# Attention and two dense layers: normalisation moved to the dense layer's input, operand splits moved to GpSimd

## The chip, the cores and the metric

The kernel runs on one core of a Trainium2 chip. A core has five engines with queues of their own: TensorE (PE in the profile; matrix products into PSUM), VectorE (DVE), ScalarE (ACT), GpSimd (POOL, which reads and writes SBUF alone) and SyncE (SP), which here issues most DMAs. The metric is the device time of the program in microseconds, lower is better.

## The reference

Block-causal attention over 4 batches x 8 heads, 576 positions, 64 channels a head, then two dense layers on 2,304 tokens of 512 channels with 2,048 hidden ones. All is float32.

```python
scores = scale * np.matmul(q, k.transpose(0, 1, 3, 2))      # scale 1/8
mask = block_i >= block_j                                   # blocks of 64 positions
scores = np.where(mask, scores, -1e9)
scores = scores - np.max(scores, axis=-1, keepdims=True)
attn = np.exp(scores)
attn = attn / (np.sum(attn, axis=-1, keepdims=True) + 1e-09)
x = np.matmul(attn, v)                                      # heads side by side: (2304, 512)
h = x @ w_in;  g = h * np.clip(h + 3.0, 0.0, 6.0) / 6.0;  x = g @ w_out
h = x @ w_in2; g = h * np.tanh(softplus(h));              out = g @ w_out2
```

## The kernel before

**Float32 in two parts.** A float32 operand x is written as hi, x stored as float32r (the format that TensorE takes at its fast rate), and lo = x - hi, stored as float32r too. A product is then two or three float32r matmuls. Making hi is a copy on some engine, making lo a subtraction of two tensors.

**A head.** q, k and v of head n are loaded by SP (`load_qk`, `load_v`), two buffers each, q and k twice, into both halves of the partitions. ScalarE makes hi of k (`split_k_hi`, L588), VectorE hi and lo of the scaled q (`split_q_hi` L781, `split_q_lo` L786) and hi and lo of v (L842, L850), GpSimd lo of k (L976). The scores of a head are five row tiles i = 0 to 4, of 128, 256, 384, 512 and 576 columns (`scores(s, i)`, L405 with hi of k, L410 with lo; L408 adds the mask to the last 64 columns; tile 0 is computed 256 wide). For each tile VectorE takes the negative row maximum (`row_max`, L792, L796), ScalarE the exponential with the row sum (`exps`, L599), VectorE the reciprocal of the sum (L799), and GpSimd multiplies the tile by it (`normalise`, L969). Then TensorE transposes the tile in 128 x 128 pieces (`prob_transposes(s, u)`, L423, four groups u = 0 to 3 in four PSUM banks), ScalarE copies the transposed pieces out as hi (`split_probs_hi`, L605 to L609) and VectorE makes lo (`split_probs_lo`, L802). Group 0 and a corner of group 3 stay in full float32 (`pt32`). `attend(s, half)` (L443) multiplies with v, [hi | lo] of v being the stationary operand: half 0 gives the first 256 positions from `pt32`, half 1 the other 320. ScalarE copies the result to SBUF (`copy_o`, L614), and SP stores it to `attn_t` in DRAM (`store_o`, L294).

**Order.** Every engine runs a list of its own, written out by hand in `attention_step`: a step works on head n, the scores of n + 1 and the q and k of n + 2. Steps 2 to 23 run in a hardware loop of two steps, the others are unrolled. Engines wait on semaphores alone.

**The seam.** `EARLY_ADD`, `EARLY_X` and `EARLY_W` name the steps in which first pieces of the dense layer are prepared: four chunks c of the first x block (`add_x` on GpSimd, L994, adds the two halves of the product; `split_x_hi` on ScalarE; `split_x_lo` on GpSimd, L998) and weight tiles 0 to 3 (`split_w_hi` on ScalarE, L670, `split_w_lo` on VectorE, L860). All four chunks are ready by step 29; SP has loaded weight tiles 4 and 5 as well (`load_w`, 512 KB each, two buffers `wraw`). In the last step TensorE puts `h_matmuls` of hidden tiles 0 and 1 between the parts of head 31 to fill its waits; then `dense_block` takes hidden tile f + 3 (`h_matmuls`) and output step f (`y_matmuls`) in turn. `h_matmuls(f)` of the first block waits for weight tile f, and the first one for all x chunks.

Of the kernel before, what the change touches and what calls it, by code (L numbers as in the profile page):

```python
# [5 lines left out]
ALU = mybir.AluOpType  # L21
# [34 lines left out]
PT_COLS = P * (4 * 4 + 4) + TAIL  # L56

PT, PL, ST, AV = 4, 3, NT, 2
FIRST, LOOP_FROM, LOOP_TO = -2, 2, NHEAD - 8


def build(nc, qk, v_main, v_tail, w, w2, out):
    ctx = ExitStack()
    with ctx:
# [8 lines left out]
        x2_t = nc.dram_tensor("x2_t", (D, TOK), F32).ap()  # L73

# [4 lines left out]
        xraw = [sb(f"xraw{s}", [P, 2, TB], F32) for s in range(2)]  # L79
# [20 lines left out]
        rowsum = [sb(f"rowsum{s}", [P, NT], F32) for s in range(2)]  # L100
        rinv = [sb(f"rinv{s}", [P, NT], F32) for s in range(2)]

        with ExitStack() as att:
# [10 lines left out]

            pt32 = [ab(f"pt32{s}", [P, 3 * P + TAIL], F32) for s in range(2)]
# [21 lines left out]

        q_hi = sem("q_hi")
# [9 lines left out]
        rinv_ready = sem("rinv_ready")  # L148
        probs_ready = sem("probs_ready")
# [4 lines left out]
        p_lo = sem("p_lo")  # L154

# [8 lines left out]
        x_added = sem("x_added")  # L164
        x_hi = sem("x_hi")
# [51 lines left out]
        def count(step, ahead, m, c):  # L217

            g, par = step
            return g * (2 * m) + ((par + ahead) * m + c)  # L220

        def slot(step, ahead):
            return (step[1] + ahead) % 2

        def has(step, ahead):

            g, par = step
            return not isinstance(g, int) or 0 <= 2 * g + par + ahead < NHEAD

        def pairs(step, ahead):  # L230

            g, par = step
            return g + ((par + ahead) // 2 + 1)

        def steps(n0, n1):
            return [(n // 2, n % 2) for n in range(n0, n1)]

        SCORE_BANK = (0, 2, 0, 1, 2)
        PT_BANK = (3, 4, 5, 6)
# [8 lines left out]
        def early(table, step):  # L253

            g, par = step
            return table.get(2 * g + par, ()) if isinstance(g, int) else ()


        def pt_source(u):

            w = P if u < 3 else TAIL
            return bank(PT_BANK[u], (u + 2) * w).rearrange("p (j q) -> p j q", q=w)[:, 0:min(u + 2, 4), :]

        def pt_part(t, u):

            i = u + 1
            if i < 4:
                return t[:, i * P:i * P + (i + 1) * 4 * P].rearrange("p (j q) -> p j q", q=4 * P)[:, :, 0:P]
            return t[:, 4 * P:20 * P].rearrange("p (j q) -> p j q", q=4 * P)[:, :, 0:TAIL]
# [3 lines left out]
        def _(sp):  # L273
            def load_qk(step, ahead):

                if has(step, ahead - 2):
                    sp.wait_ge(q_lo, count(step, ahead - 2, 1, 1))
                    sp.wait_ge(k_lo, count(step, ahead - 2, 1, 1))
                s, n = slot(step, ahead), count(step, ahead, 1, 0)
                for half in range(2):  # L280
                    sp.dma_start(qkin[s][half * DH:(half + 1) * DH, :, :], qk[n, :, :, :]).then_inc(qk_loaded[s], 16)

            def load_v(step, ahead):
                if has(step, ahead - 2):
                    sp.wait_ge(v_split, count(step, ahead - 2, 1, 1))
# [17 lines left out]
            def load_x(layer, blk, c):  # L303

                if not (blk == (0, None) and c < 2):
                    sp.wait_ge(x_lo, lin(blk, DC, c - 1))
# [755 lines left out]
```

## Time and profile before

| | |
|---|---|
| time, median of 3 runs | 1075.72 us (1075.23 to 1076.01) |
| span of the profiled execution, first to last instruction | 1073.4 us |
| TensorE busy | 1026.8 us, 96% |
| VectorE busy | 723.4 us, 67% |
| ScalarE busy | 551.4 us, 51% |
| GpSimd busy | 266.0 us, 25% |
| mean granted TensorE clock | 0.996 of full |

The profiled execution has no time of its own beside its span; the runs of the table were timed separately. Busy shares are means over a kernel with two very different parts, the attention (up to about 265 us) and the dense layers. A group of instructions lists busy time, mean length in ns and the idle time of the engine ahead of it with the engine that ended it. Lengths of instructions back to back on VectorE overlap a little, so a sum of lengths is more than the busy time.

### The profile page before, as it was taken

Reading aid. Unit: us, or ns where it says so; the run is one execution under the profiler, and the core shown is the slowest. Engines: PE = TensorE matmul, PEld = TensorE weight load, DVE = VectorE, ACT = ScalarE, POOL = GpSimd, SP = SyncE. Lnnn points to the kernel's source line nnn. Section 1 sums busy time; section 2 is a strip of 40 time slices with the busy share of each in tenths; the row PEclk is TensorE's granted clock in tenths of the full one; section 3 lists DMA queues with packets and bytes.
Section 4 is the critical chain, followed back from the end, with each engine's and each line's share of the span. In section 5 each row is a group of like instructions: output and inputs, shape, how many; then the busy total and the mean of one; then the engine's idle time right before and its main releaser. Section 6 shows DMA issues by size and latency. Waiting matters only on the chain.

```text
span 1073.4 us, 18142 instructions
## 1 busy us (share of the span) xinstructions
PE 1026.8 (96%) x5760; PEld 952.7 (89%) x5760; DVE 723.4 (67%) x1468; ACT 551.4 (51%) x1257; POOL 266.0 (25%) x275
## 2 busy tenths in 40 slices
PE   4889898988999999999999999999999999999998
PEld 3777777778999999999999999898999989999896
DVE  5999999995732223222232356988988889888886
ACT  5777787876632223222232345655555555555553
POOL 3777777795210202002020010010100001000000
PEclk9999999999999999999999999999999999999999
DMA  6656555652621101111011143200001000010000
GB/s 183 177 133 143 129 145 135 171 146 73 194 69 45 45 1 59 29 44 44 0 59 54 51 134 127 68 16 30 24 7 44 15 29 23 6 44 0 30 1 30
DMA packets 38087, 73.92 MB, mean 69 GB/s; under 512 B 7072, under 2 KB 23456, under 8 KB 38048
## 3 DMA queue, kind: packets, MB, share of 16 engines
q1 hardware_dynamic: 32000, 63.98, 21.9%
q10 hardware_dynamic: 6048, 9.44, 2.4%
q8 instruction: 22, 0.36, 0.1%
q14 instruction: 17, 0.14, 0.0%
HBM read 54.53 MB, written 18.87 MB: 68 GB/s over the span
## 4 chain that ended last, share of the span: by engine, by line
PE 75%; DVE 16%; issue 6%; POOL 1%; ACT 1%; DMA 0%; DVEq 0%; SPq 0%
PE psum L534 36%; PE psum L511 12%; PE psum L510 12%; PE psum L509 12%; DVE negmax L792 3%; DVE qs L786 2%; DVE wlo_early L802 2%; DVE rinv L799 1%; DVE ptlo L802 1%; DVE negmax L796 1%; DVE qs L781 1%; DVE vs L842 1%; DVE vs L850 1%; PE psum L443 1%; POOL klo L976 1%
## 5 line engine op out<-in xcount | busy, mean ns | idle before, releaser
L998 POOL TENSOR_TENSOR xlo<-xraw,xhi 128x384 f32 (+1 forms) x48 | 58.7, 1222 | 640.8 <-ACT xhi L679 640.8
L906 DVE SCALAR_TENSOR_TENSOR gbuf<-ebuf,psum 128x384 f32<-128x384 f32 x96 | 53.1, 553 | 230.5 <-ACT ebuf L731 230.5
L731 ACT ACTIVATE ebuf<-psum,three 128x384 f32<-128x384 f32 x96 | 55.8, 581 | 246.4 <-PE psum L511 246.4
L969 POOL TENSOR_TENSOR prob<-prob,rinv 128x128 f32<-128x128 f32 (+4 forms) x160 | 140.1, 892 | 62.7 <-DVE rinv L799 62.7
L511 PE MATMUL psum<-xhi,wlo_late 128*128 (+1 forms) x384 | 129.9, 338 | 0.0
L510 PE MATMUL psum<-xlo,whi_late 128*128 (+1 forms) x384 | 129.8, 338 | 0.0
L509 PE MATMUL psum<-xhi,whi_late 128*128 (+1 forms) x384 | 129.5, 337 | 0.0
L509 PE MATMUL psum<-xhi,whi_early 128*128 (+1 forms) x384 | 128.7, 335 | 0.0
L511 PE MATMUL psum<-xhi,wlo_early 128*128 (+1 forms) x384 | 128.7, 335 | 0.0
L510 PE MATMUL psum<-xlo,whi_early 128*128 (+1 forms) x384 | 128.5, 335 | 0.0
L704 ACT ACTIVATE ghi<-gbuf 128x384 fp32r<-128x384 f32 x192 | 100.1, 522 | 54.8 <-DVE gbuf L927 53.5
L873 DVE SCALAR_TENSOR_TENSOR glo<-gbuf,ghi 128x384 fp32r<-128x384 f32 x192 | 121.9, 635 | 4.2 <-ACT ghi L704 3.6
L599 ACT ACTIVATE prob<-psum,negmax 128x128 f32<-128x128 f32 (+4 forms) x160 | 91.2, 572 | 51.0 <-DVE negmax L796 37.7
L405 PE MATMUL psum<-khi,qs 128*128 128x256 f32 (+2 forms) x192 | 75.5, 398 | 40.9 <-ACT prob L599 24.1
L738 ACT ACTIVATE late<-ebuf,two 128x384 f32<-128x384 f32 x96 | 59.2, 616 | 87.9 <-DVE ebuf L890 87.8
L405 PEld LDWEIGHTS psum<-khi,qs 128*128 128x128 f32 x192 | 37.9, 197 | 51.6 <-ACT prob L599 29.1
L423 PE MATMUL psum<-ident,prob 128*128 128x128 f32 x480 | 73.7, 279 | 0.5 <-POOL prob L969 0.5
L510 PEld LDWEIGHTS psum<-xlo,whi_late 128*128 128x128 f32 x384 | 72.1, 188 | 2.3
L509 PEld LDWEIGHTS psum<-xhi,whi_late 128*128 128x128 f32 x384 | 72.1, 188 | 2.1
L510 PEld LDWEIGHTS psum<-xlo,whi_early 128*128 128x128 f32 x384 | 72.1, 188 | 2.0
L509 PEld LDWEIGHTS psum<-xhi,whi_early 128*128 128x128 f32 x384 | 72.1, 188 | 1.9
L410 PE MATMUL psum<-klo,qs 128*128 128x256 f32 (+2 forms) x192 | 72.9, 385 | 0.0
(92 smaller groups left out, 2587.3 us busy)
## 6 DMA issues: line engine op xcount, KB each, us to landing
qkin<-in_qk SPq DMA_DIRECT2D x64, 288.0 KB, 4.3
wraw<-in_w SPq DMA_DIRECT2D x32, 512.0 KB, 3.4
attn_t<-late SPq DMA_DIRECT2D x64, 144.0 KB, 2.4
xraw<-attn_t SPq DMA_DIRECT2D x24, 384.0 KB, 3.3
x_t<-ystage ACTq DMA_DIRECT2D x24, 192.0 KB, 1.9
xraw<-x_t SPq DMA_DIRECT2D x24, 192.0 KB, 2.4
out<-ystage ACTq DMA_DIRECT2D x18, 256.0 KB, 2.1
vin<-in_v_main SPq DMA_DIRECT2D x32, 128.0 KB, 2.5
```

What stands on the lines that cost most here:

```text
L405: pe.matmul(bank(pb, w), q_tile, khi[s][:, k0:k0 + w], start=True, stop=False)
L410: last = pe.matmul(bank(pb, w), q_tile, klo[s][:, k0:k0 + w], start=False, stop=True)
L423: last = pe.transpose(bank(PT_BANK[u], P, c0), prob[s][:, POFF[i] + j * P:POFF[i] + (j + 1) * P], ident[:, :])
L509: pe.matmul(bank(f % HB, TB), hi, x_part(xhi, blk, c), start=(c == 0), stop=False)
L510: pe.matmul(bank(f % HB, TB), hi, x_part(xlo, blk, c), start=False, stop=False)
L511: last = pe.matmul(bank(f % HB, TB), lo, x_part(xhi, blk, c), start=False, stop=(c == DC - 1))
L534: last = pe.matmul(bank(4 + c, Y_COLS[layer]), stat, mov, start=(f == 0 and m == 0), stop=(f == FT - 1 and m == 2), skip_group_check=True)
L599: nc.scalar.activation(dst, src, ACT.Exp, bias=negmax[s][:, i:i + 1], accum_out=rowsum[s][:, i:i + 1]).then_inc(exp_done, 1)
L704: nc.scalar.activation(ghi[f % GS][:, :], gbuf[f % 2][:, :], ACT.Copy, scale=(1.0 / 6.0 if layer == 0 else 1.0)).then_inc(g_hi, 1)
L738: nc.scalar.activation(rbuf[f % 2][:, :], ebuf[f % 2][:, :], ACT.Ln, bias=two[:, 0:1]).then_inc(ln_ready, 1)
L873: nc.vector.scalar_tensor_tensor(out=glo[f % GS][:, :], in0=gbuf[f % 2][:, :], scalar=(1.0 / 6.0 if layer == 0 else 1.0), in1=ghi[f % GS][ ...
L969: nc.gpsimd.tensor_tensor(p, p, rinv[s][:, i:i + 1].to_broadcast([P, w]), ALU.mult).then_inc(probs_ready, 1)
```

## The change

1. **Normalisation.** The probabilities stay unnormalised. Row sums of the eight heads of a batch are gathered in one tile; at the end of a batch TensorE transposes it (`turn_sums`), VectorE takes the reciprocals (`invert_sums`), SP stores them to DRAM (`store_rinv`, five DMAs). `load_x` of the first dense layer fetches with every x chunk the reciprocals, each row broadcast to 64 partitions (two more DMAs), and `add_x` gets a second operation on GpSimd that multiplies by them.
2. **q, k, v on GpSimd.** It scales q in place, makes hi of k, q and v by copies, and lo of q, v and k by subtractions, for q and k three heads ahead. ScalarE and VectorE no longer touch them. `copy_o` moves from ScalarE to VectorE.
3. **Transposed probabilities.** All are kept in two float32r parts; `pt32` goes. `attend` is 2 matmuls of 128 columns in half 0 and 10 of 448, 320, 192 and 64 columns in half 1. Score tile 0 is computed 128 wide.
4. **Order.** Everything is unrolled from step -3, with a new interleaving, other PSUM banks for the scores (two pairs by the parity of the head) and other steps for the early work; SP loads weight tiles 2 and 3 at step 4 and tile 4 only after the last stores.

```diff
-PT_COLS = P * (4 * 4 + 4) + TAIL
+PT_ROW = SEQ - P
+PT_COLS = (NT + 1) * PT_ROW
+PT_ORDER = (0, 1, 3, 2)
+FIRST = -3
...
-        EARLY_ADD = {NHEAD - 8: (0,), NHEAD - 7: (1,), NHEAD - 5: (2,), NHEAD - 4: (3,)}
-        EARLY_X = {NHEAD - 7: (0,), NHEAD - 6: (1,), NHEAD - 4: (2,), NHEAD - 3: (3,)}
-        EARLY_W = {-2: (0, 1), -1: (2, 3)}
+        EARLY_ADD = {NHEAD - 5: 0, NHEAD - 4: 1, NHEAD - 3: 2, NHEAD - 2: 3}
+        EARLY_X = {NHEAD - 4: 0, NHEAD - 3: 1, NHEAD - 2: 2, NHEAD - 1: 3}
+        EARLY_W = {-2: 0, -1: 1, NHEAD - 2: 2, NHEAD - 1: 3}
...
+            def store_rinv(b):
+                sp.wait_ge(rinv_ready, b + 1)
+                for i in range(NT):
...
+                    sp.dma_start(r_d[:, t0 + i * P:t0 + i * P + w], rinv[i * HEADS:(i + 1) * HEADS, 0:w]
+                                 ).then_inc(rinv_stored, 16)
...
+                    for h in range(2):
+                        sp.dma_start(x[h * DH:(h + 1) * DH, 2, :],
+                                     r_d[2 * c + h:2 * c + h + 1, tokens].to_broadcast([DH, TB])
...
+                if in_use(n):
+                    store_o(n)
+                    if n % HEADS == HEADS - 1:
+                        store_rinv(n // HEADS)
+            for f in range(4, FT):
...
                 load_w(0, f)
+            attention_stored(BATCH)
...
             def attend(n, half):
...
+                    parts = [(0, 0, t[s][:, 0:P]) for t in (pthi, ptlo)]
...
+                    parts = [(j, max(j - 1, 0) * P, pt_row(t[s], j, max(j, 1) * P))
+                             for j in range(NT) for t in (pthi, ptlo)]
...
             def attention_step(n):          # TensorE
+                last_step = n == NHEAD - 1
+                if in_use(n + 1):
+                    scores(n + 1, 2)
+                if in_use(n):
+                    prob_transposes(n, 3)
+                if in_use(n + 1):
+                    scores(n + 1, 3)
+                if in_use(n):
+                    prob_transposes(n, 2)
                 if last_step:
                     h_matmuls((0, None), 0)
+                if in_use(n + 1):
+                    scores(n + 1, 4)
+                if in_use(n):
+                    attend(n, 0)
                 if last_step:
                     h_matmuls((0, None), 1)
+                if in_use(n + 2):
+                    scores(n + 2, 0)
+                if in_use(n + 1):
+                    prob_transposes(n + 1, 0)
+                    prob_transposes(n + 1, 1)
+                if in_use(n + 2):
+                    scores(n + 2, 1)
+                if in_use(n):
+                    attend(n, 1)
+                    if n % HEADS == HEADS - 1:
+                        turn_sums(n // HEADS)
...
+            def attention_step(n):          # VectorE
+                if in_use(n):
+                    split_probs_lo(n, 3)
+                    copy_o(n, 0)
+                    split_probs_lo(n, 2)
+                if in_use(n + 1):
+                    row_max(n + 1, 4)
+                if in_use(n + 2):
+                    row_max(n + 2, 0)
+                if in_use(n + 1):
+                    split_probs_lo(n + 1, 0)
+                if in_use(n + 2):
+                    row_max(n + 2, 1)
+                if in_use(n):
+                    copy_o(n, 1)
+                if in_use(n + 2):
+                    row_max(n + 2, 2)
+                if in_use(n + 1):
+                    split_probs_lo(n + 1, 1)
+                if in_use(n + 2):
+                    row_max(n + 2, 3)
+                if n in EARLY_W:
+                    split_w_lo(0, EARLY_W[n])
+                if in_use(n) and n % HEADS == HEADS - 1:
+                    invert_sums(n // HEADS)
...
+            def attention_step(n):          # GpSimd
+                if in_use(n + 3):
+                    scale_q(n + 3)
+                    split_k_hi(n + 3)
+                    split_q_hi(n + 3)
+                if in_use(n + 1):
+                    split_v_hi(n + 1)
+                if in_use(n + 3):
+                    split_q_lo(n + 3)
+                if in_use(n + 1):
+                    split_v_lo(n + 1)
+                if in_use(n + 3):
+                    split_k_lo(n + 3)
+                if n in EARLY_ADD:
+                    add_x((0, None), EARLY_ADD[n])
+                if n in EARLY_X:
+                    split_x_lo(0, (0, None), EARLY_X[n])
...
                 nc.gpsimd.tensor_tensor(x[:, 0, :], x[:, 0, :], x[:, 1, :], ALU.add).then_inc(x_added, 1)
+                pool.wait_ge(x_added, lin(blk, DC, c + 1))
+                nc.gpsimd.tensor_tensor(x[:, 0, :], x[:, 0, :], x[:, 2, :], ALU.mult).then_inc(x_scaled, 1)
```

## Rows read from the trace of the kernel before

**Rows 1.** Head of the page of the profile.

```profile
span 1073.4 us, 18142 instructions
```

**Rows 2.** Windows: length, busy us (count) of PE, PEld, DVE, ACT, POOL; clock, DMA.

```profile
60.00:210.60 150.60, 134.34 (x905) 113.28 (x902) 149.34 (x341) 118.75 (x361) 114.76 (x121) 1.00 0.59 142
...
248.00:251.00 3.00, 2.77 (x11) 2.70 (x12) 0.82 (x4) 1.15 (x5) 2.77 (x5) 0.53 0.03 5
...
300.00:400.00 100.00, 100.00 (x573) 100.00 (x572) 28.10 (x52) 28.90 (x57) 10.57 (x10) 1.00 0.12 38
```

**Rows 3.** Groups by line, VectorE, 60 to 210.6 us (20 heads).

```profile
L792 DVE TENSOR_REDUCE negmax<-psum 128x1 f32<-128x256 f32 (+1 forms) x80 | 36.5, 477 | 0.0
...
L781 DVE TENSOR_SCALAR qs<-qkin 128x576 fp32r<-128x576 f32 x21 | 25.6, 1219 | 0.0
...
L786 DVE SCALAR_TENSOR_TENSOR qs<-qkin,qs 64x576 fp32r<-64x576 f32 x20 | 25.1, 1256 | 0.6
...
L799 DVE RECIPROCAL rinv<-rowsum 128x1 f32<-128x1 f32 x100 | 15.3, 153 | 0.6
...
L802 DVE TENSOR_TENSOR ptlo<-psum,pthi 128x384 fp32r<-128x384 f32 (+2 forms) x30 | 14.7, 544 | 0.0
...
L850 DVE TENSOR_TENSOR vs<-vin,vs 128x320 fp32r<-128x320 f32 x20 | 13.7, 683 | 0.0
...
L842 DVE CAST vs<-vin 128x320 fp32r<-128x320 f32 x20 | 9.3, 465 | 0.0
```

**Rows 4.** Groups by line, GpSimd, 60 to 210.6 us.

```profile
L969 POOL TENSOR_TENSOR prob<-prob,rinv 128x512 f32<-128x512 f32 (+4 forms) x101 | 89.5, 902 | 35.8 <-DVE rinv L799 35.8
...
L976 POOL TENSOR_TENSOR klo<-qkin,khi 128x576 fp32r<-128x576 f32 x20 | 28.1, 1406 | 0.0
```

**Rows 5.** Groups by form, GpSimd, 0 to 30 us.

```profile
L969 POOL TENSOR_TENSOR prob<-prob,rinv 128x576 f32<-128x576 f32 x1 | 1.1, 1141 | 0.0
...
L1014 POOL TENSOR_SCALAR_AFFINE_SELECT ident<-ident 128x128 f32<-128x128 f32 x1 | 0.3, 292 | 0.2 <-POOL two L1012 0.2
...
L1008 POOL MEMSET ident<- 128x128 f32 x1 | 0.2, 204 | 0.3 <-POOLq L1049 0.3
...
L1011 POOL MEMSET three<- 128x1 f32 x1 | 0.1, 98 | 0.0
```

**Rows 6.** Timeline, VectorE, before GpSimd is at work.

```profile
6.08 0.46 DVE L781 TENSOR_SCALAR qs<-qkin 128x576 fp32r<-128x576 f32 x1 [4.03 <-DMA qkin<-in_qk]
```

**Rows 7.** Timeline, TensorE: start us, length us; brackets: idle time, releaser.

```profile
27.77 0.41 PE L443 MATMUL psum<-whi_early,vs 128*128 128x320 f32 x1
...
40.71 0.81 PE L443 MATMUL psum<-pt,vs 128*128 128x256 f32 x4
...
42.34 0.38 PE L405 MATMUL psum<-khi,qs 128*128 128x256 f32 x1 [0.81 <-ACT prob L599]
...
248.23 0.55 PE L405 MATMUL psum<-khi,qs 128*128 128x256 f32 x1 [2.28 <-POOL klo L976]
...
262.62 0.42 PE L509 MATMUL psum<-xhi,whi_early 128*128 128x384 f32 x1
...
264.79 0.31 PE L443 MATMUL psum<-pthi,vs 128*128 128x320 f32 x1
...
266.13 0.34 PE L509 MATMUL psum<-xhi,whi_early 128*128 128x384 f32 x1
...
270.43 0.44 PE L534 MATMUL psum<-ghi,whi_early 128*128 128x384 f32 x1
```

**Rows 8.** Timelines of ScalarE, VectorE, SP; DMA issues of the weight tiles.

```profile
272.88 1.06 ACT L670 ACTIVATE whi_early<-wraw 128x1024 fp32r<-128x1024 f32 x1 [1.99 <-DMA wraw<-in_w]
...
273.97 1.23 DVE L860 TENSOR_TENSOR wlo_early<-wraw,whi_early 128x1024 fp32r<-128x1024 f32 x1 [1.53 <-ACT whi_early L670]
...
266.79 1.12 SPq L294 DMA_DIRECT2D attn_t<-late  x2
...
wraw<-in_w SPq DMA_DIRECT2D x32, 512.0 KB, 3.4
```

More of the change, by code:

```diff
@@ L272, in _, with pt_row @@
+            if u == 0:
+                return rows[:, 0:3, 0:P]
+            return rows[:, 1:u + 3, u * P:u * P + (P if u < 3 else TAIL)]
+        def pt_row(t, j, q0):
+            return t[:, PT_ROW * (j + 1) + q0 - P:PT_ROW * (j + 2)]
         @block.sync
         def _(sp):
[L274 to L279, printed above, removed]
-                for half in range(2):
-                    sp.dma_start(qkin[s][half * DH:(half + 1) * DH, :, :], qk[n, :, :, :]).then_inc(qk_loaded[s], 16)
@@ L283, in load_v, with load_qk @@
[L283 to L295 removed]
+            def load_qk(n):
+                if in_use(n - 2):
+                    sp.wait_ge(q_lo, n - 1)
+                    sp.wait_ge(k_lo, n - 1)
+                for half in range(2):
+                    sp.dma_start(qkin[n % 2][half * DH:(half + 1) * DH, :, :], qk[n, :, :, :]
+                                 ).then_inc(qk_loaded[n % 2], 16)
@@ L323, in _ @@
-            for step in steps(-2, LOOP_FROM):
-                load_qk(step, 4)
-                if has(step, 1):
-                    load_v(step, 3)
-                if not has(step, 1):
+            load_qk(0)
+            load_w(0, 0)
+            load_qk(1)
+            load_v(0)
+            load_w(0, 1)
+            load_v(1)
+            for n in range(FIRST, NHEAD):
+                if 2 <= n + 5 < NHEAD:
+                    load_qk(n + 5)
+                if 2 <= n + 3 < NHEAD:
+                    load_v(n + 3)
+                if n == 4:
@@ L328, in _ @@
                     load_w(0, 2)
                     load_w(0, 3)
-                if has(step, 0):
-                    store_o(step, 0, step[1])
-            load_w(0, 4)
-            load_w(0, 5)
-            with sp.Fori(LOOP_FROM // 2, LOOP_TO // 2) as g:
-                batch, pair = sp.snap(g // (HEADS // 2)), sp.snap(g % (HEADS // 2))
-                for par in range(2):
-                    load_qk((g, par), 4)
-                    load_v((g, par), 3)
-                    store_o((g, par), batch, pair * 2 + par)
@@ L494, in attention_step @@
-                if has(step, 0):
-                    pe.wait_ge(p_lo, count(step, 0, PL, 3))
-                    attend(s0, 1)
+                if in_use(n + 2):
[9 more added lines that the diff above has]
+                        turn_sums(n // HEADS)
```

500 lines of the change are left out of this document (196 added, 304 removed).

## The prediction

> **What bounds the kernel now.** The profiled execution spans 1073.4 us [rows 1]; the median of the runs is 1075.7, so 2.3 us lie around the span, and I carry them over unchanged. I read the stretches first. In a stretch of dense work TensorE is busy for all of its 100 us [rows 2], and I take the dense layers to be like it throughout: no helper engine sets their time. In the attention loop (20 heads in 150.6 us, 7.53 us a head) it is another picture: VectorE is busy for 149.3 of the 150.6 us, TensorE for 134.3, GpSimd 114.8, ScalarE 118.8 [rows 2]. So VectorE sets the period of the 32 heads, and TensorE pays with one gap of about 0.8 us a head, waiting for an exponential that waits for a row maximum [rows 7]. Next comes VectorE's own list [rows 3] and GpSimd's [rows 4], since the change empties the first and fills the second. Last the seam between attention and dense layer [rows 7, 8]. Measured from the first second-half `attend` (27.77) to the last (264.79) less the two `h_matmuls` put between (2.17 each, as the one from 262.62), the 31 periods take 237.0 - 4.3 = 232.7 us [rows 7].
>
> **VectorE.** Removed per head: the two q splits (25.6/21 + 25.1/20 = 2.48), five reciprocals (0.77), the v cast and v remainder (0.47 + 0.68): 4.4 us. Kept: four row maxima (36.5/20 = 1.83) and the fifth, of 576 columns (0.74, an estimate from the remainder's 0.54 for 384), and three remainders (0.54 each) [rows 3]. Added: a remainder of 384 columns (0.54), 64 columns more in the tail's (0.07), two copies out of PSUM of 128 and 448 columns (about 0.28 and 0.61, as PSUM reads of such width in these rows). Sum 5.7 us as listed, an upper bound, since back-to-back instructions overlap a little in the records. VectorE is no longer the bound.
>
> **ScalarE** was busy for 5.9 us a head [rows 2]. It loses the k cast and both copies of the output, keeps the exponentials and gets no new operation in the loop (the first transposed tile becomes float32r, the tail's two copies one), so it stays under 5.9 and is not the bound.
>
> **GpSimd.** Removed: five normalisations, 89.5/20 = 4.5 us a head. Kept: k remainder, 1.41 [rows 4]. Added: `scale_q`, `split_k_hi`, `split_q_hi` (one input, 576 columns), `split_v_hi` (one input, 320), `split_q_lo` (two inputs, 576 columns on half of the partitions; the time goes by columns, 1.4), `split_v_lo` (two inputs, 320: 1.41 x 320/576 and a fixed part, 0.87). Nothing in the trace is a one-input copy or scale on GpSimd. Bounds for 576 columns: from below the memsets, 0.10 for one column and 0.20 for 128, so 0.8 ns a column, 0.10 + 0.45 = 0.56; from above the multiply with a broadcast operand that the profile has undisturbed, 1.14. The one op with one tensor input, the select that makes the identity, took 0.29 for 128 columns: 0.19 above the one-column memset, 1.5 ns a column, 0.96 at 576 [rows 5]. I take 0.90, nearest to that row, and 0.53 for 320 columns. Sum: 3 x 0.90 + 0.53 + 2 x 1.41 + 0.87 = 6.9, less 0.04 overlap for each of seven, 6.65; by the bounds 5.6 and 7.4. The Trainium skill says of GpSimd (GPSIMD Engine Reference, 4.1 Engine selection) that one-input ops run roughly at line rate; by that, an estimate of 0.5 plus a fixed 0.15, the head would cost GpSimd about 5.9. The same page (8. Key points) calls VectorE about twice as fast for elementwise work, which speaks against moving the splits; no run here has the one-input case.
>
> GpSimd did not run free before: with it busy, VectorE's `split_q_hi` took 1.22 us [rows 3], alone 0.46 [rows 6]. After the change every VectorE operation of the loop reads PSUM, with at most one operand in SBUF, the kind that kept its 0.54 us beside a busy GpSimd [rows 3]. So I add no contention. The Trainium skill has the rule (SBUF — State Buffer, Who interferes with whom): VectorE contends with GpSimd in two-port modes or with two SBUF inputs, not otherwise; the pair 0.46 and 1.22 agrees.
>
> **TensorE.** A head holds 7.53 less the gap of 0.8, 6.7 us of matmuls, of it 0.2 the end of the last one ahead of the gap: 6.5. `attend` took about 0.6 for 384 columns in full float32 (0.8 with its end) and 1.34 for the second half (264.79 to 266.13) [rows 7]. Now it is twelve float32r matmuls with 3,200 columns (2 x 128 in the first half; 4 x 448, 2 x 320, 2 x 192, 2 x 64 in the second). One `h_matmuls`, twelve float32r matmuls of 384 columns, takes 2.17 us [rows 7], 0.47 ns a column, so 1.5 for all; the narrow ones cannot follow each other quite so fast, and I take 1.7 against 1.94. The first score tile is 128 wide, not 256: 256 columns less, -0.1. That gives 6.1 us. But matmuls in float32r under 256 columns (128, 192, 64 and the 128-wide scores, 768 + 256 columns a head) do not occur before. The bound from above: they cost what full float32 costs, 0.81 us for 384 columns [rows 7]; with 0.2 taken off for the end of the last one, 1.6 ns each, so 1,024 x (1.6 - 0.47) ns = 1.2 us more, less the allowance for narrow ones: 7.2 us. I take the float32r row, the nearest in kind.
>
> **Period.** GpSimd's 6.65 is the longest of the sums as taken, before TensorE's 6.1, ScalarE's under 5.9 and VectorE's 5.7. Each head has to go through TensorE, ScalarE and VectorE in turn, and I add 0.15 for waits between engines this close: 6.8. The new order gives each chain (scores, maximum, exponential, transpose, split, remainder) half a head or more before TensorE asks for it, and q, k and v are made up to three heads ahead, so I find no chain of the loop longer than the period. SP gets no new DMA inside a batch; its loads of q and k wait for GpSimd's remainders two heads back and land in 4 us, under a head. 31 x 6.8 = 210.8: -21.9 us.
>
> **Start.** GpSimd now makes q and k of head 0 in five operations one after another, 3 x 0.9 + 2 x 1.4 = 5.5 us against 2.7 before, but two of the four early weight splits leave ScalarE's and VectorE's start (1.06 and 1.23 each [rows 8]). I count 0, bounds -2 and +3.
>
> **Seam.** Two new waits. First, the last early x chunk is now split in the last step, after `prob_transposes(31, 2)`: ScalarE's split of 512 columns of probabilities and of 384 of x (0.6 and 0.5, from its 1.06 for 1,024), GpSimd's remainder (1.0 for 384 columns, by the 1.41 for 576 [rows 4]), and the hand-overs 0.1: `h_matmuls(0)` stands 2.2 us on TensorE, and behind it, in order, both halves of `attend`. Second, SP: weight tiles 4 and 5 were loaded ahead, so TensorE had no gap from 262.62 to the first y at 270.43 (two `h_matmuls` of 2.17 after `attend`) [rows 7]. Now `load_w(0, 4)` stands behind `store_o(31)` and `store_rinv(3)`. From the end of the last `attend`: copy and inversion about 0.6, seven issues at 0.56 (two took 1.12), issue and landing of the tile 3.4, ScalarE 1.06, VectorE 1.23 [rows 8]: about 10.2 us. TensorE has h(2), h(3) and y(0) to do, 3 x 2.17: it waits 3.7 us for tile 4. Such gaps have a second price: after 2.28 us of idleness the 3 us from 248 ran at a granted clock of 0.53, the 1.2 GHz level [rows 2, 7], where work takes twice its time: +1.5 us a gap. Against that, part of the first gap only takes the place of waits that the last step had before. I take the two waits as 5.6 (of 5.9) and the clock as 0.7: seam +6.3. With no new wait it would be 0; with both at the lower clock and slower small loads, 10.
> The store of the inverses, the broadcast loads and the extra multiply (one of 1.0 us for each of 24 chunks) lie in the dense layer beside TensorE's full load, where GpSimd is busy a tenth of the time [rows 2]; four batch ends add a 128-column transpose and a reciprocal of some 0.3 us, hidden. If that cover went, 24 us.
>
> **Sum.** 1073.4 - 21.9 + 0 + 6.3 + 2.3 = 1060 us.
>
> **Rivals.**
> A. Copies on GpSimd near memset rate (0.7 an operation or less, so GpSimd at most 5.9) and narrow float32r at full rate: 6.1 a head, bound by TensorE, 189.1 - 232.7 + 6.3: 1038, and 1032 if TensorE's sum is too high by 0.2. For it: the memset rows [rows 5]. Against: no tensor is read in them. The line-rate rule of the Trainium skill named above would give this case.
> B. Narrow float32r costs like float32: TensorE 7.2 a head, 223.2 us, -9.5 + 6.3: 1072. For it: full float32 at 1.6 against 0.47 ns a column shows how much a fall-back would cost. Against: no row shows one.
> C. The other side: one-input operations cost what the broadcast multiply does, 1.14, or more. GpSimd then needs 7.4 a head, 7.5 with the waits between engines, as much as VectorE needed before; the loop gives back nothing, and the seam stays: 1082. It decides from a period of 7.3, where the loop's gain equals the seam: GpSimd at 7.15, an operation at 1.04. At 1.41, the two-input price, a head takes 8.6 and the kernel 1116.
> D. The loop is as said and the seam costs nothing, the new waits hidden by work that moves up: 1054.
>
> **Chances.** As said, with D (1052 to 1066): 0.46. A: 0.17. B: 0.15. C: 0.22, of it 0.04 within 0.2% of before (2.2 us, about what a measurement of this kernel can tell from no change). Faster 0.78, same 0.04, slower 0.18. A range of 1032 to 1084 leaves out the far ends of A and C; the likeliest case by itself has 1052 to 1067.
>
> **What would show it.** GpSimd busy above 0.9 in the loop, VectorE near 0.75; heads 6.8 us apart; the three 576-column operations near 0.9; TensorE's waits on `q_lo`/`k_lo`; a gap of 2 us before the first `h_matmuls`, one of 4 before h(4), ended by a weight remainder. It is wrong if a one-input operation takes over 1.04 us, if matmuls of 64 to 192 columns take more than 0.15, or if GpSimd's q and k come late for the scores although it has idle time.

## The result and the profile after

The changed kernel takes 1082.05 us (median of 6 runs, 1079.91 to 1084.32), the kernel before 1075.87 on the same chip (6 runs, 1073.87 to 1078.49): ratio 1.0056, 95% interval 1.0041 to 1.0071. It is slower by 0.6%; the forecast was 1060 and faster. The profiled execution spans 1082.5 us, is the longest of the six (1084.32 by its own time) and ran at a mean granted clock of 0.982 (before: 0.996), so a ledger made on it has 9.1 us to explain where the medians differ by 6.2.

The head of the page after, with its busy shares and the chain that ended last by engine:

```profile
span 1082.5 us, 16881 instructions
...
PE 1012.1 (94%) x5700; PEld 947.0 (87%) x5700; DVE 661.9 (61%) x1278; ACT 511.4 (47%) x1129; POOL 331.0 (31%) x331
...
PE 77%; POOL 11%; issue 5%; DVE 3%; DMA 3%; SPq 1%; ACT 0%; POOLq 0%; DVEq 0%
```

The same chain before:

```profile
PE 75%; DVE 16%; issue 6%; POOL 1%; ACT 1%; DMA 0%; DVEq 0%; SPq 0%
```

GpSimd has taken VectorE's place on the chain, and 3% of it are now DMAs. The windows after, with the columns of [rows 2], answer to them; the stretch from 100 to 150 and two short ones are added:

```profile
60.00:210.00 150.00, 125.58 (x877) 110.26 (x875) 110.00 (x227) 95.37 (x285) 139.93 (x143) 0.98 0.58 149
100.00:150.00 50.00, 42.24 (x301) 37.00 (x300) 37.53 (x78) 32.62 (x98) 47.94 (x50) 1.00 0.58 145
72.00:76.00 4.00, 0.00 (x0) 0.00 (x0) 0.92 (x3) 0.05 (x1) 3.71 (x6) 0.83 0.96 253
76.00:80.00 4.00, 3.97 (x14) 3.53 (x15) 2.26 (x5) 1.64 (x6) 2.99 (x2) 0.50 0.35 94
...
300.00:400.00 100.00, 100.00 (x579) 100.00 (x578) 33.45 (x55) 32.08 (x61) 22.34 (x21) 1.00 0.23 71
```

From 100 to 150 GpSimd is busy for 47.94 of 50 us and nobody else is near: the loop is bound where the forecast put it. But the second-half `attend` of successive heads starts every 7.20 us, not every 6.8. GpSimd's forms after say why (60 to 210 us; busy, mean ns, idle before):

```profile
L881 POOL TENSOR_SCALAR qkin<-qkin 128x576 f32<-128x576 f32 x20 | 33.2, 1658 | 0.0
L903 POOL TENSOR_TENSOR qs<-qkin,qs 64x576 fp32r<-64x576 f32 x21 | 29.8, 1417 | 3.2 <-POOL vs L917 2.6
L909 POOL TENSOR_TENSOR klo<-qkin,khi 128x576 fp32r<-128x576 f32 x21 | 29.6, 1409 | 0.0
L923 POOL TENSOR_TENSOR vs<-vin,vs 128x320 fp32r<-128x320 f32 x21 | 18.3, 873 | 3.0
L888 POOL CAST qs<-qkin 128x576 fp32r<-128x576 f32 x20 | 13.5, 675 | 0.0
L894 POOL CAST khi<-qkin 128x576 fp32r<-128x576 f32 x20 | 13.4, 670 | 4.0 <-PE psum L397 4.0
L917 POOL CAST vs<-vin 128x320 fp32r<-128x320 f32 x20 | 9.2, 461 | 0.0
```

The seven means sum to 7.16 us. In 100 to 150 GpSimd is busy for 6.90 us a head (47.94/50 of 7.20): back-to-back instructions overlap by about 0.04 each in the records, and the other 0.29 us of the period are two waits of GpSimd on itself. `split_q_lo` (L903) and `split_v_lo` (L923) each wait for a semaphore that the instruction right before them in GpSimd's own list raises: 3.2 us in 21 and 3.0 in 21, 0.15 and 0.14 a head. The three remainders are as forecast (1.42, 1.41, 0.87). The casts are cheaper than the 0.90 and 0.53 taken: 0.67 and 0.46. The scaling of q in place (L881) is far dearer: 1.66, more than a subtraction with two inputs.

The short windows show a second loss. In 72 to 76 TensorE does nothing and the DMA engines are 0.96 busy; in 76 to 80 it works at 0.50, the 1.2 GHz level. SP's queue and VectorE's timeline around that place, after:

```profile
64.89 0.47 SPq L262 DMA_DIRECT2D vin<-in_v_tail  x1
65.39 1.06 SPq L289 DMA_DIRECT2D wraw<-in_w  x2
66.50 1.27 SPq L268 DMA_DIRECT2D attn_t<-late  x2
```

```profile
75.08 0.29 DVE L743 COPY late<-psum 128x128 f32<-128x128 f32 x1 [6.16 <-DMA attn_t<-late]
75.29 0.68 DVE L734 TENSOR_TENSOR wlo_early<-psum,whi_early 128x512 fp32r<-128x512 f32 x1
75.89 0.75 DVE L729 TENSOR_REDUCE negmax<-psum 128x1 f32<-128x576 f32 x1
```

In step 4 SP issues two weight tiles (1 MB) and then `store_o(4)`. The second half of the store lands at 74.99, 8.0 us after its issue; in the other steps a half takes 3.1 (median). `copy_o(6)` wants the stage buffer of head 4, so it stands on VectorE for 6.16 us, and behind it, in order, stand the remainder of the probabilities (L734) and the row maximum (L729), for which TensorE and ScalarE wait in turn. At step 26 VectorE waits in the same way, 4.70 us up to 236.16, but for another reason: six DMAs of the x chunks stand ahead of `store_o(26)`, and SP needs 3.5 us to issue them. The store then lands 3.9 us after its own issue, not 8. SP's queue there, after:

```profile
227.98 0.52 SPq L298 DMA_DIRECT2D xraw<-attn_t  x1
...
231.50 1.23 SPq L268 DMA_DIRECT2D attn_t<-late  x2
```

TensorE's waits at the seam, after, and ScalarE's queue there (the counterparts of [rows 7, 8]):

```profile
261.82 0.69 PE L485 MATMUL psum<-xhi,whi_early 128*128 128x384 f32 x1 [4.31 <-POOL xlo L954]
...
280.79 0.69 PE L510 MATMUL psum<-ghi,whi_early 128*128 128x384 f32 x1 [5.93 <-DVE glo L794]
```

```profile
277.49 1.06 ACT L616 ACTIVATE whi_early<-wraw 128x1024 fp32r<-128x1024 f32 x1 [10.88 <-DMA wraw<-in_w]
278.45 0.56 ACT L677 ACTIVATE ebuf<-psum,three 128x384 f32<-128x384 f32 x1
278.92 0.51 ACT L650 ACTIVATE ghi<-gbuf 128x384 fp32r<-128x384 f32 x1
```

The first wait is for x chunk 3. Its buffer is freed by the remainder of chunk 1 only at 253.4, the chunk and its reciprocals land at 257.7, then four GpSimd operations of 1.0 follow: the chunk's two, and behind them the remainders of chunk 2 and of chunk 3. After the wait TensorE works at the 1.2 GHz level: the granted clock is 0.52 in 262 to 266, and `h_matmuls(0)` takes 4.0 us (261.82 to 265.83) instead of 2.17. GpSimd's timeline, after:

```profile
257.80 0.99 POOL L948 TENSOR_TENSOR xraw<-xraw 128x384 f32<-128x384 f32 x1 [3.11 <-DMA xraw<-r_d]
258.87 0.99 POOL L950 TENSOR_TENSOR xraw<-xraw 128x384 f32<-128x384 f32 x1
259.82 1.95 POOL L954 TENSOR_TENSOR xlo<-xraw,xhi 128x384 fp32r<-128x384 f32 x2
```

The second wait is not at h(4), as forecast, but at the first `y_matmuls`: ScalarE's queue holds `split_w_hi(4)` ahead of `split_g_hi` of the first hidden tile, and stands in it for 10.88 us until the late tile 4 has landed.

Where the time went, in the profiled executions (marks: start of second-half `attend` of head 0, of head 31, first `y_matmuls`, end; before: 27.77, 264.79, 270.43, 1073.4 [rows 1, 7]; after: 28.71, 268.14, 280.79, 1082.5):

| part | after less before, us |
|---|---|
| start, up to head 0 | +0.9 |
| 31 periods of 7.20 for 7.506 | -9.5 |
| heads 6 to 9 take 32.9 for 28.8 (store behind two weight tiles) | +4.1 |
| heads 28 to 30 take 25.0 for 21.6 (store behind six x DMAs, x work) | +3.4 |
| last step, 16.1 for 7.2 + 4.3 (wait for x chunk 3) | +4.6 |
| last `attend` to the first y, 12.65 for 5.64 (weight tile 4) | +7.0 |
| dense layers | -1.3 |
| sum (remainder -0.1 to the spans' +9.1) | +9.2 |

The last step is set against a full period and the two `h_matmuls`. But the last heads have less to do: where all early work is done ahead (e6 below) heads 30 and 31 take 5.46 and 7.45 us, the two `h_matmuls` included. Against that the waits of the last step cost 8.7 us, not 4.6.

### The profile page after: what moved, and what is told of

It is laid out like the page before. It is cut to its first block, busy times and chain, and to the rows that moved or that the text cites. A ratio compares the mean times of both kernels' runs of the same rounds, so it can differ in the third digit from the quotient of the medians.

```text
span 1082.5 us, 16881 instructions
## 1 busy us (share of the span) xinstructions
PE 1012.1 (94%) x5700; PEld 947.0 (87%) x5700; DVE 661.9 (61%) x1278; ACT 511.4 (47%) x1129; POOL 331.0 (31%) x331
## 4 chain that ended last, share of the span: by engine, by line
PE 77%; POOL 11%; issue 5%; DVE 3%; DMA 3%; SPq 1%; ACT 0%; POOLq 0%; DVEq 0%
PE psum L510 36%; PE psum L485 12%; PE psum L487 12%; PE psum L486 12%; POOL qkin L881 3%; POOL qs L903 3%; PE psum L435 2%; POOL vs L923 2%; POOL qs L888 1%; PE psum L415 1%; DMA xraw<-r_d 1%; PE psum L397 1%; PE psum L392 1%; POOL vs L917 1%; DMA attn_t<-late 1%
## 5 line engine op out<-in xcount | busy, mean ns | idle before, releaser
L392 PE MATMUL psum<-khi,qs 128*128 128x128 f32 (+2 forms) x192 | 73.0, 385 | 38.3 <-issue 24.0
L725 DVE TENSOR_REDUCE negmax<-psum 128x1 f32<-128x128 f32 (+3 forms) x128 | 62.3, 486 | 22.1 <-PE psum L397 18.8
L487 PEld LDWEIGHTS psum<-xhi,wlo_early 128*128 128x128 f32 x384 | 72.9, 190 | 0.0
```

Source lines behind the costliest of these rows:

```text
L392: pe.matmul(bank(pb, w), q_tile, khi[s][:, k0:k0 + w], start=True, stop=False)
L487: last = pe.matmul(bank(f % HB, TB), lo, x_part(xhi, blk, c), start=False, stop=(c == DC - 1))
L725: nc.vector.reduce_max(negmax[s][:, i:i + 1], bank(b, PW[i]), AX.X, negate=True).then_inc(max_ready, 1)
```

## Experiments

Each run of a kernel of its own is set against runs of the kernel before on the same chip, as a ratio with a 95% interval. "Period" is the distance of second-half `attend`s in steps without extra work. Four suspects: the scaling operation, the store behind the weight tiles, the x chunks, weight tile 4.

**e1, stores first.** In each step SP issues `store_o` ahead of the weight tiles and of the x chunks of the first block; nothing else is changed.

```diff
+                if in_use(n):
+                    store_o(n)
                 if n == 4:
                     load_w(0, 2)
                     load_w(0, 3)
...
-                if in_use(n):
-                    store_o(n)
```

> Only SP's order differs from the changed kernel: in steps 4, 26, 28 and 29 the store of the head's output is issued before the two weight tiles and the x chunks, not behind them. Theory 1 (the store of head 4 and head 26 lies in the DMA queues behind 1 MB of other loads, and copy_o two heads later waits for its buffer): the two long periods of 11.6 and 10.1 us fall to about 7.2, and the periods around them lose their slow-clock tail; the span falls by 6 to 7.5 us, to about 1075. Rival (the DMA engines are simply full there, whoever comes first): the wait moves to the loads of q, k, v of the next heads, GpSimd idles, and less than 3 us come back.

Measured: 1080.41 us, ratio 1.0053 (1.0037 to 1.0070), span 1078.1. Heads 6 to 9 are back at 7.20 each: the store behind the weight tiles is shown as the cause there. At the x chunks the wait only moved. GpSimd's and TensorE's timelines of this kernel:

```profile
229.62 1.01 POOL L948 TENSOR_TENSOR xraw<-xraw 128x384 f32<-128x384 f32 x1 [2.09 <-DMA xraw<-r_d]
230.71 0.99 POOL L950 TENSOR_TENSOR xraw<-xraw 128x384 f32<-128x384 f32 x1
231.67 1.65 POOL L881 TENSOR_SCALAR qkin<-qkin 128x576 f32<-128x576 f32 x1
```

```profile
233.79 0.69 PE L392 MATMUL psum<-khi,qs 128*128 128x384 f32 x1 [3.16 <-ACT prob L574]
```

The x DMAs, now issued later, are late for `add_x`; GpSimd stands, ScalarE's x split waits for it with the exponentials behind, and TensorE waits 3.16 us. Head 29 takes 11.7 us and the last step 18.0 instead of 16.1. So the expectation held for one half: the span fell by 4.4 us, not by 6 to 7.5, and the median by 1.6.

**e2, weights ahead.** Weight tiles 2 and 3 are split in steps 8 and 10 instead of 30 and 31, which frees their buffers, and tiles 4 and 5 are loaded in step 12.

```diff
-        EARLY_W = {-2: 0, -1: 1, NHEAD - 2: 2, NHEAD - 1: 3}
+        EARLY_W = {-2: 0, -1: 1, 8: 2, 10: 3}
+                if n == 12:
+                    load_w(0, 4)
+                    load_w(0, 5)
...
-            for f in range(4, FT):
+            for f in range(6, FT):
```

> Weight tiles 2 and 3 are split in steps 8 and 10 instead of 30 and 31, and SP loads tiles 4 and 5 in step 12, behind the store. Theory 1 (the 5.9 us gap ahead of the first y is the load of tile 4, which SP issues only after the last stores, and ScalarE's queue stands behind its split): the gap goes, with its slow-clock tail; 6 to 8 us less than the changed kernel, about 1075. Rival (the gap belongs to the store of the reciprocals and the wait for the inverted sums ahead of the dense block): it stays at 5 us or more, and less than 2 us come back.

Measured: 1074.63 us (10 runs), ratio 0.9989 (0.9974 to 1.0004), span 1075.7. TensorE's timeline of this kernel at the seam:

```profile
263.88 0.69 PE L488 MATMUL psum<-xhi,whi_early 128*128 128x384 f32 x1 [6.24 <-POOL xlo L957]
...
276.65 0.34 PE L513 MATMUL psum<-ghi,whi_early 128*128 128x384 f32 x1
```

The first y has no wait any more: from the last `attend` (270.84) to it 5.81 us instead of 12.65, which is [rows 7]'s 5.64 again. Some of the 6.8 is paid back in the loop (heads 9 and 11 take 7.7 and 8.2, the wait for chunk 3 is 6.24 for 4.31), some more is won in the dense layers (2.7 us). Against the changed kernel the medians give -7.4 us, as expected. The late weight tile is shown as the cause of the wait at the first y, and its price there is the ledger's. Heads 9 and 11 show a price of weight splits in the loop. VectorE's and GpSimd's timelines of this kernel:

```profile
95.21 1.97 DVE L784 TENSOR_TENSOR wlo_early<-wraw,whi_early 128x1024 fp32r<-128x1024 f32 x1
```

```profile
96.07 2.62 POOL L884 TENSOR_SCALAR qkin<-qkin 128x576 f32<-128x576 f32 x1
```

VectorE's remainder of a weight tile, with both inputs in SBUF, runs for 1.97 us where it takes 1.22 elsewhere, and GpSimd's scaling beside it for 2.62 instead of 1.66. The same happens again at 110 us.

**e3, scaling on ScalarE.** `scale_q(n + 4)` goes to ScalarE, behind `exps(n + 1, 3)`, as one activation; GpSimd keeps the rest.

```diff
-                nc.gpsimd.tensor_scalar(q, q, SCALE, None, ALU.mult).then_inc(q_scaled, 1)
+                nc.scalar.activation(q, q, ACT.Copy, scale=SCALE).then_inc(q_scaled, 1)
```

> The scaling of q (1.66 us a head on GpSimd) is done by ScalarE in place, with one Copy with scale, a step ahead; nothing else moves. Theory 1 (GpSimd's sum is the period of the loop): GpSimd needs 5.5 us a head, TensorE becomes the bound at 6.2 to 6.5, 0.7 to 1.0 us a head less: 22 to 31 us less than the changed kernel, 1051 to 1060. Rival (the chain of TensorE, ScalarE and VectorE is as long as the period already): less than 5 us.

Measured: 1129.49 us, ratio 1.0498 (1.0479 to 1.0516), span 1127.6. The expectation failed badly. The waits of this kernel in 60 to 210 us (total, times, longest):

```profile
POOL khi L898 <- PE psum L397: 61.3, 12, 7.5
...
PE psum L392 <- ACT prob L579: 39.4, 9, 4.9
ACT qkin L562 <- DMA qkin<-in_qk: 36.0, 8, 4.9
```

The scaling itself costs ScalarE 0.68 us. But the q and k of head n + 4 are loaded only when GpSimd has used up those of n + 2, and they had not landed; ScalarE stood up to 4.9 us in the scaling with the exponentials behind it, TensorE waited for them, GpSimd waited for the scores, and so loaded later still. Heads alternate between 11.3 to 13.9 and about 5.8 us, and over 60 to 210 us the granted clock is 0.85.

**e4, scaling as a multiply with a broadcast operand.** The same shape in place, but as the two-input operation with a one-column tile of 1/8.

```diff
-                nc.gpsimd.tensor_scalar(q, q, SCALE, None, ALU.mult).then_inc(q_scaled, 1)
+                nc.gpsimd.tensor_tensor(q, q, eighth[:, 0:1].to_broadcast([P, SEQ]), ALU.mult).then_inc(q_scaled, 1)
```

> GpSimd keeps the scaling, but as a multiply of two tensors whose second is one broadcast column, the form that took 1.14 us for 576 columns before. Theory 1 (GpSimd bounds the loop, and its tensor_scalar is slow as an instruction, not because it writes in place): the operation takes 1.14 instead of 1.66, the period 6.7 instead of 7.2, 15 to 16 us less: about 1066. Rival (in-place work over the whole tile is what costs, in any form): it takes about 1.66 again and the time is that of the changed kernel, within 3 us.

Measured: 1069.32 us, ratio 0.9940 (0.9923 to 0.9957), span 1069.7. The operation takes 1.15 us, the period is 6.67, as expected. The stalls are at the same places as in the changed kernel, and in the loop and the last step longer: head 6 takes 12.8 us (VectorE's wait for the store is 7.42 for 6.16), and heads 6 to 9, heads 28 to 30 and the last step stand 7.3, 4.3 and 5.4 us above the period, where they stood 4.1, 3.4 and 4.6. These 4.9 us account for the shortfall: 12.7 us came back, and not 15 to 16. With this one line the change is faster than before, by 0.6%. The operation's row in this kernel:

```profile
L882 POOL TENSOR_TENSOR qkin<-qkin,eighth 128x576 f32<-128x576 f32 x21 | 24.1, 1149 | 1.4 <-DMA qkin<-in_qk 1.4
```

**e5, scaling on ScalarE, later.** As e3, but `scale_q(n + 3)`, behind `exps(n + 1, 1)`.

> As the run before with the scaling of q on ScalarE, but asked for a head later in ScalarE's queue (head n + 3 in step n, behind the exponential of tile 1), so that the load has landed when ScalarE comes to it. Theory 1 (the 12 us periods of that run come from ScalarE's queue standing behind a load that waits, through the two buffers, for GpSimd; GpSimd's sum is still what bounds the changed kernel): periods of 6.2 to 6.6, the rest of the ledger as in the changed kernel, 22 to 31 us less than it: 1051 to 1060. Rival (two q and k buffers can't feed a loop shorter than 7 us, or the chain of TensorE, ScalarE and VectorE is as long): 7.0 us or more a head, above 1072.

Measured: 1053.61 us (1050.79 to 1059.31), ratio 0.9796 (0.9750 to 0.9842), span 1054.4, inside the expected 1051 to 1060. Periods go from 5.65 to 7.5, 6.3 on average from head 10 to head 27. ScalarE still waits for loads in the scaling, 8.3 us in all from 100 to 150 and 2.3 at most at once, but no longer long enough to start the alternation. The stalls at head 6 and at the seam are there as before.

**e6, the work of the seam ahead.** Stores first; weight tiles 2 to 5 loaded one at a time in steps 4, 6, 19, 21 and tiles 2, 3 split in 8 and 10; the four x chunks loaded in 11, 13, 16, 18, added in 14, 16, 20, 22 and split a step later; the next block's two in the last steps. GpSimd keeps its 1.66 us scaling.

```diff
-        EARLY_ADD = {NHEAD - 5: 0, NHEAD - 4: 1, NHEAD - 3: 2, NHEAD - 2: 3}
-        EARLY_X = {NHEAD - 4: 0, NHEAD - 3: 1, NHEAD - 2: 2, NHEAD - 1: 3}
-        EARLY_W = {-2: 0, -1: 1, NHEAD - 2: 2, NHEAD - 1: 3}
+        EARLY_ADD = {14: 0, 16: 1, 20: 2, 22: 3}
+        EARLY_X = {15: 0, 17: 1, 21: 2, 23: 3}
+        EARLY_W = {-2: 0, -1: 1, 8: 2, 10: 3}
+        LOAD_W = {4: 2, 6: 3, 19: 4, 21: 5}
+        LOAD_X = {11: 0, 13: 1, 16: 2, 18: 3}
```

> Scaling as in the changed kernel. Stores first in each step of SP; weight tiles 2 to 5 one at a time in steps 4, 6, 19 and 21; x chunks one at a time in steps 11 to 18, made in steps 14 to 23; so none of this is left for the end. Theory 1 (the ledger: 4.1 us at heads 6 to 9, 3.4 at 28 to 30, 4.6 in the last step, 7.0 between the last attend and the first y): all four go, and GpSimd, the bound, pays for 12 us of x work in the loop: 1082 - 19 + 8 to 12, so 1071 to 1075. Rival (these gaps are one mechanism's symptoms and come back elsewhere): above 1078.

Measured: 1070.62 us, ratio 0.9955 (0.9938 to 0.9971), span 1067.6, just under the expected 1071 to 1075. Every stall of the ledger is gone: head 6 at 7.19, last step 7.45 with both `h_matmuls`, 5.8 from the last `attend` to the first y. But steps with early work take up to 10.2 us. Heads 16 to 24 come to 12.0 us above 7.2 a head, the 12 x 1.0 us of GpSimd that the four chunks need; heads 9 to 12, beside the two weight splits, come to 2.0, and two GpSimd operations there are 1.0 us longer than usual, as in e2. Where GpSimd sets the period, its x work is paid in full.

**e7 and e8, both remedies together.** e6's schedule with e4's multiply, and with e5's scaling on ScalarE.

> Work ahead, and q scaled on GpSimd by the broadcast multiply. Theory 1: 0.53 us a head less than the run with work ahead alone, -16: 1055 to 1060. Rival: as soon as the loop is shorter, ScalarE and VectorE chains bound it, less than 8 us less.

> Work ahead, and q scaled by ScalarE where the load has landed. GpSimd has 5.5 us a head, TensorE 6.2: x work on GpSimd is hidden. Theory 1: periods 6.2 to 6.5, no gaps at the end, 1036 to 1046. Rival: ScalarE or the chain bounds at 7: above 1060.

Measured: e7 1054.08 us, ratio 0.9801 (0.9779 to 0.9823), period 6.67; e8 1036.57 us, ratio 0.9635 (0.9607 to 0.9662), span 1034.5, periods 5.65 to 8.2; e7 is 1 us under what was expected, e8 at its lower end. Against the changed kernel e4 saves 12.7 us, e6 11.4 and both together 28.0, 3.9 more than the sum. The ledgers have a reason for it: the faster loop of e4 made the stalls 4.9 us longer, and in e7 they are not there. The medians alone, from several chips, would not settle a difference of this size.

**e9, a copy in place.** The changed kernel with the scaling replaced by a copy onto the same place; the scaling is left out.

```diff
-                nc.gpsimd.tensor_scalar(q, q, SCALE, None, ALU.mult).then_inc(q_scaled, 1)
+                nc.gpsimd.tensor_copy(q, q).then_inc(q_scaled, 1)
```

> The changed kernel with GpSimd's scaling of q replaced by a plain copy onto the same place, same shape (so q stays unscaled: the scaling by 1/8 is left out). It tells apart two reasons for the 1.66 us: that the operation writes where it reads, or that it is arithmetic with a constant instead of a copy. Theory (the kind of instruction): the copy in place takes 0.67 us like the two casts, GpSimd's list falls from 7.16 to about 6.2 a head, the loop is then bound by TensorE or near it at about 6.3 (31 x 0.9 less, so a span near 1056 with the stalls of the changed kernel left in). Rival (writing in place): the copy takes about 1.6 too and the span stays at 1080.

Measured: 1052.51 us, ratio 0.9792 (0.9769 to 0.9815), span 1049.7, period 6.18. The row of this kernel:

```profile
L881 POOL COPY qkin<-qkin 128x576 f32<-128x576 f32 x23 | 15.3, 664 | 0.0
```

0.66 us, with tensor and place unchanged: it is not the writing in place that costs 1.66, it is the operation with a constant. GpSimd's list is now 6.17 us, and the period 6.18: from 100 to 200 us GpSimd has no idle time but the two short waits on itself, so it still sets the period, and not TensorE, as had been expected.

**e10, no scaling of q.** e6's schedule; the exponential takes the scale 1/8, and VectorE multiplies each negated row maximum by 1/8.

```diff
-                nc.scalar.activation(dst, src, ACT.Exp, bias=negmax[s][:, i:i + 1],
+                nc.scalar.activation(dst, src, ACT.Exp, scale=SCALE, bias=negmax[s][:, i:i + 1],
+                nc.vector.tensor_scalar(negmax[s][:, i:i + 1], rawmax[s][:, i:i + 1], SCALE, None, ALU.mult
+                                        ).then_inc(max_ready, 1)
```

> The schedule of e8, but q is not scaled at all: the exponential takes scale 1/8, and VectorE multiplies each negated row maximum by 1/8 (an operation of 128x1, five a head). GpSimd's list is then 5.5 us a head, ScalarE has no operation that waits for a load, and VectorE gets five small operations of about 0.1 to 0.15 us (0.5 to 0.75 us on a list of 5.4). Theory: the loop is bound by TensorE, 6.1 to 6.4 a head without the uneven periods of e8 (mean 6.5), which gives a span of 1025 to 1032. Rival: the extra operation stands on the chain from scores to exponential, TensorE waits for it, and the period is 6.5 or more, no better than e8's 1034.5.

Measured: 1032.76 us (1032.63 to 1033.06), ratio 0.9598 (0.9582 to 0.9614), span 1031.0, granted clock 1.00. Its windows and the row of the new operation:

```profile
100.00:150.00 50.00, 46.22 (x331) 41.25 (x330) 45.03 (x124) 37.59 (x110) 46.82 (x54) 1.00 0.76 196
```

```profile
L730 DVE TENSOR_SCALAR negmax<-rawmax 128x1 f32<-128x1 f32 x115 | 17.7, 154 | 3.9
```

In steps without extra work the period is 5.85. Steps with x work and those after them take 6.1 to 8.1; VectorE, GpSimd and TensorE are all busy for 0.9 or more of this stretch. Which of them sets the period here is not shown. It is the fastest kernel here: 4.0% less than before, and it has everything that the change set out to do except GpSimd's scaling and the late loads.

## Why the forecast was wrong

Each term of the forecast beside what the profiled executions showed:

| term | forecast | measured |
|---|---|---|
| loop, 31 periods | -21.9 (6.8 each) | -9.5 (7.20 each) |
| DMAs inside the loop (heads 6 to 9, 28 to 30) | 0 | +7.5 |
| seam (last step, first y) | +6.3 | +11.6 |
| start | 0 | +0.9 |
| dense layers | 0 | -1.3 |

**The price of the one-input operations on GpSimd failed**, the step that said "I take 0.90". It put one price on `scale_q`, `split_k_hi` and `split_q_hi`, because all have one tensor input. The copies took 0.67 and the operation with a constant 1.66. Three at 0.90 are 2.70, the real three 3.00; with the cheaper cast of v the seven came to 7.16 instead of 6.92, 7.4 us over 31 heads. e4 (1.15, period 6.67) and e9 (0.66, period 6.18) show that the period follows this one operation. Rival C had the right kind of failure, a one-input price above 1.04. That its time, 1082, is the measured one is luck: C's loop gives back nothing and its seam costs 6.3, while the measured loop gave back 9.5, DMAs inside it took 7.5 and the seam 11.6. No operation took 1.14, and 1.66 lies outside the bounds, which ended at the two-input price of 1.41. (C's 7.4 raises the three operations of 576 columns alone; with the cast of 320 columns raised too it is 7.5, and C's time 1087.) The row used for the estimate, the select of 128 columns at 0.29 [rows 5], is an operation with arithmetic and lies between copy and scaling; taking it as the price of both hid that they differ.

**The allowance around GpSimd's list failed as well.** The forecast took 0.28 off for overlap and put 0.15 on for waits between engines. The overlap came, the waits between engines did not; the two waits of GpSimd on its own semaphores, 0.29 a head, were not in the sum. So the period is 0.04 above the sum of the seven, and not 0.12 below it: 5.0 us over 31 heads. With the 7.4 of the prices these are the 12.4 us that the loop was off.

Of the copies the Trainium skill's rule (GPSIMD Engine Reference, 4.1 Engine selection), one-input operations at roughly line rate, is borne out: 0.46 us at 320 columns and 0.67 at 576, 0.8 ns for each further column, and VectorE's cast of 320 columns took 0.47 too [rows 3]. For the operation with a constant it does not hold; the measured 1.66 decides.

**"SP gets no new DMA inside a batch" failed.** It is wrong by the diff itself: weight tiles 2 and 3 had moved into step 4, and the x loads of steps 26 and 28 had grown from one DMA a chunk to three and stood ahead of the store. The forecast put this term at nothing. It asked only whether loads come in time, and not whether a store behind them frees its buffer in time. e1 shows the first place (heads 6 to 9 back at 7.20). For the second, e6 takes the gap away, and e1 shows that the order alone does not. The loop's 12.4 us alone would have left the change faster than before (1060 + 12.4 is 1072); with the 7.5 us here and 5.3 more at the seam it is slower. All terms together give 1084.8, the profiled execution's own 1084.3. After each such stop TensorE also worked at the 1.2 GHz level for some microseconds (0.50 in 76 to 80), as [rows 2, 7] had shown for another gap; the forecast charged that to the seam alone.

**The seam was right in kind and too small.** Both waits came. The first, for x chunk 3, was 4.31 us for 2.2: the forecast started its sum at the probabilities, while the chunk's load began only when the buffer of chunk 1 was free, and chunk 2's remainder stood in GpSimd's list ahead of chunk 3's. The second came to 5.93 for 3.7 and at another place: weight tile 4 was late as worked out, but the wait was not passed on through h(4). It went through ScalarE, whose queue holds the tile's split ahead of the first hidden tile's; the forecast named what is queued on TensorE and SP, not on ScalarE. So the first y could not fill the wait: 3.7 and its 2.17 are 5.9. The lower clock, taken as 0.7 for both gaps, cost 1.8 in `h_matmuls(0)` alone; the clock after the second gap (0.50 in 280 to 284, 0.71 in 284 to 288) lies in the row of the dense layers. e2 takes tile 4's part away (5.81 from `attend` to y) and leaves the other.

**A term that was missing:** the x chunks' third operation. The multiply by the reciprocals was costed for the dense layers, where it is hidden, but the four early chunks lie in the loop, where GpSimd is the bound; e6 pays for them in full (12.0 us in heads 16 to 24), e10 pays 8.8 of the 12 there, the changed kernel a part, since in its last three steps GpSimd has no more q and k to prepare.

**What held.** VectorE is no longer the bound: 37.5 of 50 us, 5.4 a head for 5.7. ScalarE 4.7 a head, under 5.9. TensorE's narrow float32r matmuls are far from the price of full float32, so rival B is out. Its timeline after:

```profile
155.59 0.37 PE L435 MATMUL psum<-ptlo,vs 128*128 128x448 f32 x1
155.80 0.31 PE L435 MATMUL psum<-pthi,vs 128*128 128x320 f32 x1
155.95 0.31 PE L435 MATMUL psum<-ptlo,vs 128*128 128x320 f32 x1
156.09 0.25 PE L435 MATMUL psum<-pthi,vs 128*128 128x192 f32 x1
156.18 0.28 PE L435 MATMUL psum<-ptlo,vs 128*128 128x192 f32 x1
156.29 0.22 PE L435 MATMUL psum<-pthi,vs 128*128 128x64 f32 x1
156.34 0.28 PE L435 MATMUL psum<-ptlo,vs 128*128 128x64 f32 x1
```

The starts are 0.21 apart for 448 columns and 0.15 for 320, 0.47 ns a column; 0.10 for 192, 0.5 ns; 0.05 for 64, 0.8 ns; the two of 128 columns in half 0 start 0.13 apart in the loop, 1.0 ns. So narrow ones cost a little more a column, as the allowance of 0.2 had it, and no narrow one takes 0.15. TensorE's 6.1 a head was slightly high; e10 runs heads of 5.85, and single heads of 5.65 occur in e1 and in e5 to e9. Two of rival A's conditions held, copies under 0.7 and cheap narrow matmuls; the scaling kept its case from coming. Its loop of about 6.1 a head fits e9. The store of the reciprocals and the broadcast loads are hidden in the dense layers, which even became 1.3 us shorter. At three batch ends `invert_sums` takes 0.94 us instead of 0.3, and TensorE waits for it for some 0.8; the periods there are 7.20 like the others, since GpSimd sets them.

What stays open: why the constant costs GpSimd a microsecond more than a copy (the runs show its price, not its cause), and how the 3.4 us of heads 28 to 30 split between the store and the x work.

## What to carry to other kernels

Before work is moved to an engine that will then set the period, price each kind of operation there by itself: copy, operation with a constant and two-input operation had three prices here (0.67, 1.66, 1.41), and leaving the costly one out (the scale in the exponential) was worth more than the new order of the early work (e10 is 37.9 us below e6, e6 11.4 below the changed kernel). An operation that waits for the one right before it on its own engine cost 0.15 us each time. For each DMA that is moved, ask what is queued behind it on its queue and in the DMA engines, stores that free a buffer above all: 1 MB of loads in front of a small store stopped VectorE for 6 us, and TensorE and ScalarE behind it. Such a stall does not shrink with the period: in the faster loop of e4 it was longer. And where an operation in an in-order queue waits for a transfer (ScalarE's weight split at the seam, its scaling in e3), its price is not its own length but that of all that stands behind it.

## What was not expected of the hardware

- GpSimd, 128x576 float32: copy or cast 0.67 us, multiply with a broadcast one-column tile 1.15, subtraction of two tensors 1.41, multiply with a constant 1.66. The same multiply takes ScalarE 0.68.
- The second of two stores of 144 KB issued right behind 1 MB of loads landed 8.0 us after its issue, the first 4.6; median in the loop 3.1, before the change 2.4.
- A multiply with a constant on GpSimd took 2.62 us instead of 1.66 beside VectorE's subtraction of 1,024 columns with both inputs in SBUF, which itself took 1.97 instead of 1.22 (e2).
- GpSimd's wait for the semaphore of its own instruction just before cost 0.14 to 0.15 us.
- A reciprocal of 40x128 from PSUM took VectorE 0.94 us; a row maximum of 576 columns took 0.75, a multiply of one column took 0.154.
- Matmuls in float32r of 192 and 64 columns start 0.10 and 0.05 us apart, 0.5 and 0.8 ns a column, against 0.47 for 320 and 448 columns.
